# Both feed-forward layers' first product by seven half-size products on two PSUM banks, with the first layer's combined weights made during tile 0

## The reference: what is computed

```python
B, H, S, D = 8, 8, 576, 64                 # q, k, v: (B, H, S, D)
k_p = k.reshape(B, H, S // 8, 8, D).mean(axis=3)      # 72 pooled keys
v_p = v.reshape(B, H, S // 8, 8, D).mean(axis=3)
attn = softmax((q @ k_p.T) / sqrt(D))
x = (attn @ v_p) laid out as (4608 tokens, 512)
h = x @ w1_in;  g = max(0.01 * h, h);               x1  = g @ w1_out
h = x1 @ w2_in; g = h * clip(h + 3, 0, 6) / 6;      out = g @ w2_out
```

## Time and profile before

| | |
|---|---|
| Time, median of 3 runs | 1769.86 us (1765.23 to 1772.93) |
| Profiled execution, its own time | 1768.24 us |
| Its span, first to last instruction | 1766.4 us |
| TensorE busy | 1723.9 us, 98% |
| VectorE, ScalarE, GpSimd busy | 896.7, 634.2, 487.8 us |
| Mean granted TensorE clock | 0.987 of full speed |
| Moved by DMA | 255.41 MB |

### The profile page before, as it was taken

How to read it: one execution, slowest core, us unless ns; L and a number is a source line. 1 busy time by engine, 2 the same in 40 slices (tenths; PEclk the granted TensorE clock), 3 DMA queues, 4 the chain that set the end, 5 groups by cost and what they waited for, 6 DMA issues and landing times.

```text
span 1766.4 us, 28990 instructions
## 1 busy us (share of the span) xinstructions
PE 1723.9 (98%) x9642; PEld 1484.3 (84%) x9642; DVE 896.7 (51%) x1498; ACT 634.2 (36%) x1161; POOL 487.8 (28%) x620
## 2 busy tenths in 40 slices
PE   7899999999999999999999799999999999999999
PEld 7787888888888888888888688998989989898898
DVE  8655555555554655653242345454545454544444
ACT  3544333333333333333222324343434333333332
POOL 7553221222221221213986413030303021121200
PEclk7899999999999999999999899999999999999999
DMA  5332122121121121214557976666756565757562
GB/s 173 112 120 76 47 66 77 45 89 61 38 87 59 63 65 45 76 45 138 189 189 255 337 275 199 198 213 187 220 177 220 178 222 173 224 173 225 174 196 76
DMA packets 141548, 255.41 MB, mean 145 GB/s; under 512 B 14528, under 2 KB 22720, under 8 KB 141504
## 3 DMA queue, kind: packets, MB, share of 16 engines
q1 hardware_dynamic: 141504, 254.86, 44.9%
HBM read 203.42 MB, written 51.38 MB: 144 GB/s over the span
## 4 chain that ended last, share of the span: by engine, by line
PE 79%; POOL 6%; DVE 6%; DMA 3%; ACT 2%; issue 2%; SPq 2%; DVEq 0%; POOLq 0%; ACTq 0%
PE ps_h L1245 14%; PE ps_y L1181 13%; PE ps_y L1183 12%; PE ps_y L1182 12%; PE ps_att L1245 6%; PE ps_h L1181 5%; PE ps_h L1183 5%; PE ps_h L1182 5%; POOL prep_stage L694 2%; PE ps_att L1181 2%; DMA prep_raw<-in_moe_w_out 2%; PE ps_att L1182 2%; PE ps_att L1183 2%; POOL prep_sum L682 2%; POOL prep_stage L692 1%
## 5 line engine op out<-in xcount | busy, mean ns | idle before, releaser
L1245 PE MATMUL ps_h<-xs_hi,ring 128*128 128x256 f32 x1440 | 301.6, 280 | 4.1 <-DMA ring<-w_in_split 3.3
L1245 PEld LDWEIGHTS ps_h<-xs_hi,ring 128*128 128x128 f32 x1440 | 240.4, 188 | 16.9 <-DMA ring<-w_in_split 3.7
L1181 PE MATMUL ps_h<-x_hi,win_hi 128*128 128x512 f32 x576 | 232.3, 403 | 6.3 <-DVE gate L997 6.3
L1181 PE MATMUL ps_y<-wout_hi,g_hi 128*128 128x512 f32 x576 | 227.0, 394 | 3.5 <-issue 3.5
L1181 PE MATMUL ps_y<-g_hi,wout_hi 128*128 128x512 f32 x576 | 229.2, 398 | 0.0
L1183 PE MATMUL ps_y<-wout_hi,g_lo 128*128 128x512 f32 x576 | 227.5, 395 | 0.0
L1183 PE MATMUL ps_h<-x_hi,win_lo 128*128 128x512 f32 x576 | 227.1, 394 | 0.0
L1182 PE MATMUL ps_h<-x_lo,win_hi 128*128 128x512 f32 x576 | 226.6, 393 | 0.0
L1183 PE MATMUL ps_y<-g_hi,wout_lo 128*128 128x512 f32 x576 | 225.9, 392 | 0.0
L1182 PE MATMUL ps_y<-wout_lo,g_hi 128*128 128x512 f32 x576 | 225.6, 392 | 0.0
L1182 PE MATMUL ps_y<-g_lo,wout_hi 128*128 128x512 f32 x576 | 225.0, 391 | 0.0
(11 more groups left out here) (134 smaller groups left out, 3144.1 us busy)
## 6 DMA issues: line engine op xcount, KB each, us to landing
ring<-w_in_split SPq DMA_DIRECT2D x504, 256.0 KB, 2.7
w_in_split<-prep_stage SPq DMA_DIRECT2D x56, 256.0 KB, 2.0
k_raw<-in_kT SPq DMA_DIRECT2D x32, 288.0 KB, 2.9
q_raw<-in_qT SPq DMA_DIRECT2D x32, 288.0 KB, 3.8
v_raw<-in_v SPq DMA_DIRECT2D x32, 288.0 KB
x0T<-x_stage SPq DMA_DIRECT2D x32, 288.0 KB, 2.1
x1T<-y_stage SPq DMA_DIRECT2D x36, 256.0 KB, 2.2
x_stage<-x1T SPq DMA_DIRECT2D x36, 256.0 KB, 3.7
```

Source lines behind the costliest of these rows:

```text
L1181: pe.matmul(acc, left[0], right[0], start=first, stop=False)
L1245: mm = pe.matmul(banks[BANK_OF[r]], a, b[:, r, c, :], start=r < 3 and c == 0 and n == 0, stop=c == 1 and n == 2, skip_group_check=True)
```

## The change

Layer 1's first product is made as layer 2's: seven products of half size per step, the factors of w1_in streamed through the same 14-slot ring in tiles 1 to 8. All 18 tiles (`ALL_TILES`) use one step form, and the first step of layer 2 follows on the last of layer 1; part of each tile's second product runs in the next tile. The seven products use two banks instead of three, in the order A11, S2, A12, S3, S1, A22, S4, so the copies and sums of one product must be done before a product two or three later opens or adds to the same bank.

Layer 1's gate is one DVE instruction that reads `h` twice from SBUF; ACT's `pre` is gone there. ACT copies 2 of a step's blocks and DVE makes 5 sums of 256 columns, in layer 1 as in layer 2. The sums and low parts of x are made on POOL in both layers.

The first layer's factors are made in tile 0, block i + 1 in step i (block 0 before it): the sums and low parts on POOL, the high parts on ACT, straight into the ring, from where SP stores them (`w1_in_split`) for the tiles after. `first_sums` and `last_x_part` make the first tile's x from the four units' results. w1_out is loaded in 8 pieces whose low parts (`piece_lo`) POOL makes in tile 0, too. In tiles 7 and 8 POOL makes 16 split rows of w2_out (`split_row`), three blocks of w2_in factors, tile 8's x, and the other five blocks, and SP stores them between its ring loads.

The order of the seven products, their banks, and the places (8 for each of a tile's 8 steps) of the attention stages in a tile:

```diff
-BANK_OF = (0, 1, 2, 0, 1, 1, 2)
+UNIT_PLACES = [(0, 3, 4, 5, 6, 9, 11, 12, 14),
+               (11, 15, 16, 17, 18, 20, 23, 24, 26),
+               (23, 27, 28, 29, 30, 33, 35, 36, 38),
+               (35, 39, 40, 41, 42, 44, 47, 48, 50)]
...
+A11, S2, A12, S3, S1, A22, S4 = range(PRODUCTS)
+B11, T2, B21, T3, T1, NT4, B22 = range(PRODUCTS)
+BANK_OF = (0, 1, 0, 1, 0, 1, 0)
+OPENS = (0, 1, 4)
...
+        banks = (ps_h[:, 0, 0:HN], ps_h[:, 1, 0:HN])
```

SyncE: tile 0, where each combined factor is stored as it is made; the loop of tiles 1 to 6; tile 7, where `rows_then_factors` stores one row of `w2_out` or one combined factor of `w2_in` at each call:

```diff
+            for i in range(HF):
+                for n in range(PRODUCTS):
+                    if i < HF - 1:
+                        store_factor(i + 1, n)
+                    if i >= HF - 2:
+                        q = PRODUCTS * i + n
+                        sp.wait_ge(ring_stored[q % RING], 16 * USES)
+                        stream(0, i, n, w1_in_split, w1_in_split)
+                    attention_at(0, HF * i + n)
+                attention_at(0, HF * i + PRODUCTS)
+                if 0 < i < HF - 2:
+                    load_raw(i + 2)
...
+            def attention_tile(T, next_unit=True):
+                for i in range(HF):
+                    for m in range(HF):
+                        for r in before_place(m):
+                            stream(T, i, r, w1_in_split, w1_in_split)
+                        attention_at(T, HF * i + m, next_unit)
+                    if i == 1:
+                        store_y(T - 1, False)
...
+            row = n = 0
+            T = ATT_TILES
             for i in range(HF):
                 for r in range(PRODUCTS):
+                    stream(T, i, r, w1_in_split, w1_in_split)
+                    if r < (2, 5, 5, 6, 6, 6, 5, 2)[i]:
+                        row, n = rows_then_factors(1, row, n)
+                if i == 0:
+                    load_x_tile(x0T, T + 1, T + 1)
```

GpSimd: the order of its whole work after the start:

```diff
+            factors(0)
+            first_sums()
+            factors(1)
             sum_unit(1, 0)
+            piece_lo(0)
+            piece_lo(1)
             sum_k(1, 1, 16)
+            factors(2)
             sum_v(1, 1, 18)
+            piece_lo(2)
+            piece_lo(3)
             sum_k(1, 2, 20)
+            factors(3)
+            factors(4)
             sum_v(1, 2, 22)
+            piece_lo(4)
+            piece_lo(5)
             sum_k(1, 3, 24)
+            factors(5)
+            piece_lo(6)
+            piece_lo(7)
             sum_v(1, 3, 26)
+            factors(6)
+            sum_k(2, 0, 28)
+            factors(7)
+            sum_v(2, 0, 30)
+            split_x(1)
+            with pool.Fori(1, ATT_TILES - 1) as T:
+                for c in range(1, PAIRS):
                     sum_unit(T + 1, c)
+                sum_unit(T + 2, 0)
+                split_x(T + 1)
+            for c in range(1, PAIRS):
+                sum_unit(ATT_TILES, c)
+            split_x(ATT_TILES)
             for e in range(FC):
+                split_row(e)
+            for i in range(3):
+                factors2(i)
+            split_x(ATT_TILES + 1)
+            for i in range(3, HF):
+                factors2(i)
+            with pool.Fori(TILES, ALL_TILES) as T:
+                split_x(T)
```

GpSimd: the low parts of one block of first-layer factors, made into the ring that TensorE reads; `factors(i)` is four sums and this:

```diff
+            def factors_lo(i):
+                for n, k in enumerate(PREP_ORDER):
+                    slot = ring_slot(PRODUCTS * i + k)
+                    pool.wait_ge(prep_hi_ready, PRODUCTS * i + n + 1)
+                    nc.gpsimd.tensor_tensor(slot[:, 2:4], factor_source(raw[:, i % 2], k),
+                                            slot[:, 0:2].bitcast(F32), ALU.subtract
+                                            ).then_inc(prep_ready, 1)
```

ScalarE: one step (`place(m)` runs the attention stages of that place, and in tile 0 one high part `factor_hi(i + 1, m)`, which for the sums waits for GpSimd):

```diff
+                act.wait_ge(product_done, PRODUCTS * s + 1)
+                above_zero(act, c21_ready, s)
+                nc.scalar.activation(p1[:], banks[0], ACT.Copy).then_inc(p1_ready, 1)
+                if i == 1 and not is_first(T):
+                    copy_y(T - 1, 0)
+                if i > 0 or not is_first(T):
+                    g_hi_of(s - 1, (i - 1) % HF, 0, before if i == 0 else layer)
+                place(0)
+                act.wait_ge(product_done, PRODUCTS * s + 3)
+                above_zero(act, gate_ready, 2 * s)
+                nc.scalar.activation(h[:, 0, 0:HN], banks[0], ACT.Copy).then_inc(c11_ready, 1)
+                if i == 1 and not is_first(T):
+                    copy_y(T - 1, 2)
+                next_x(0)
+                place(1)
+                next_x(1)
+                place(2)
+                next_x(2)
+                place(3)
+                next_x(3)
+                place(4)
+                if layer == 2:
+                    pre_of(s, 1)
+                g_hi_of(s, i, 1, layer)
+                next_x(4)
+                place(5)
+                next_x(5)
+                place(6)
+                if layer == 2:
+                    pre_of(s, 0)
+                place(7)
+                next_x(6)
```

VectorE: the first layer's gate, and one step:

```diff
+                    nc.vector.scalar_tensor_tensor(gate[:, upper], h[:, upper], SLOPE,
+                                                   h[:, upper], ALU.mult, ALU.max
+                                                   ).then_inc(gate_ready, 1)
...
+                dve.wait_ge(product_done, PRODUCTS * s + 2)
+                dve.wait_ge(p1_ready, s + 1)
+                above_zero(dve, c12_ready, s)
+                add(u2[:], 1, p1[:]).then_inc(u2_ready, 1)
+                if i > 0 or not is_first(T):
+                    last = before if i == 0 else layer
+                    gate_of(s - 1, 0, last)
+                    if is_first(T) and i == 1:
+                        dve.wait_ge(x0_stored[PAIRS - 1], 16)
+                    g_lo_of(s - 1, (i - 1) % HF, 0, last)
+                if i == 1 and not is_first(T):
+                    copy_y(T - 1, 1)
+                place(0)
+                place(1)
+                dve.wait_ge(product_done, PRODUCTS * s + 4)
+                above_zero(dve, c22_ready, s)
+                add(u3[:], 1, p1[:]).then_inc(u3_ready, 1)
+                if i == 1 and not is_first(T):
+                    copy_y(T - 1, 3)
+                place(2)
+                dve.wait_ge(product_done, PRODUCTS * s + 5)
+                dve.wait_ge(u3_ready, s + 1)
+                above_zero(dve, gate_ready, 2 * s - 1)
+                add(h[:, 1, HN:N], 0, u3[:]).then_inc(c22_ready, 1)
+                place(3)
+                dve.wait_ge(product_done, PRODUCTS * s + 6)
+                add(h[:, 1, 0:HN], 1, p1[:]).then_inc(c21_ready, 1)
+                gate_of(s, 1, layer)
+                place(4)
+                dve.wait_ge(product_done, PRODUCTS * s + 7)
+                dve.wait_ge(u2_ready, s + 1)
+                above_zero(dve, gate_ready, 2 * s)
+                add(h[:, 0, HN:N], 0, u2[:]).then_inc(c12_ready, 1)
+                place(5)
+                g_lo_of(s, i, 1, layer)
+                place(6)
+                place(7)
```

TensorE: what a product (`part`) waits for, and one step (`lagging(back, upper, j)` is a quarter, three 512-column matmuls, of the second product of the step `back` before):

```diff
+                if is_first(T):
+                    pe.wait_ge(prep_ready, PRODUCTS * i + PREP_AT[r] + 1)
+                else:
+                    pe.wait_ge(ring_loaded[q % RING], 16 * (USES * (T - 1) + q // RING + 1))
+                if i == 0 and is_first(T):
+                    first_x_ready(r)
+                elif i == 0:
+                    pe.wait_ge(x_ready, PRODUCTS * (T - 1) + r + 1)
...
+                    pe.wait_ge((p1_ready, u2_ready, c11_ready, u3_ready, c22_ready)[r - 2], s + 1)
...
+                part(T, i, 0)
+                part(T, i, 1)
+                lagging(2, 0, 2)
+                place(0)
+                part(T, i, 2)
+                lagging(2, 0, 3)
+                place(1)
+                part(T, i, 3)
+                lagging(1, 1, 0)
+                place(2)
+                part(T, i, 4)
+                lagging(1, 1, 1)
+                place(3)
+                part(T, i, 5)
+                lagging(1, 1, 2)
+                place(4)
+                part(T, i, 6)
+                lagging(1, 1, 3)
+                place(5)
+                lagging(1, 0, 0)
+                place(6)
+                lagging(1, 0, 1)
+                place(7)
```

More of the change, by code:

```diff
@@ L935, in stage, with step, place @@
                                          ACT.Copy, scale=V_SCALE).then_inc(x0_copied, 1)
-            def tile(T, attention, last=False, pieces={}):
-                for place in range(4 * FC):
-                    if place % 4 == 1:
-                        chain(T, place // 4)
+            def step(T, i, layer, before=None, attention=False, turns=True):
+                s = HF * T + i
+                before = before or layer
+                opened = is_first(T) and i == 0
+                def place(m):
@@ L1004, in copy_y, with gate_of @@
[L1004 to L1014 removed]
+            def gate_of(s, upper, layer):
@@ L1079, in spread, with add @@
+            def add(to, bank, other):
+                return nc.vector.tensor_tensor(to, banks[bank], other, ALU.add)
             def spread(per_row):
```

1310 lines of the change are left out of this document (609 added, 701 removed), and 4 rows, old and new, of the table FIRST_STAGES.

## The result

The changed kernel takes 1833.1 us (median of 4 runs, 1829.6 to 1834.7) against 1770.6: ratio 1.0355, 95% interval 1.0327 to 1.0383. It is 59 us above the forecast and outside its range. The page, part 1, to be read against the earlier trace rows: TensorE is busy 2.8 us longer than before and idle 62 us longer; GpSimd is busy 198 us longer.

What follows compares the result with a forecast made beforehand. TensorE, busy 98% of the span, sets the time. Tile 1's start 181, attention tiles 644.4, eleven tiles 924 plus 2.2, seam 10, leftover second product 6.8 and tail 3.4 give 1771.8; with 1.84 outside, 1774 us, range 1748 to 1794.

Steps and rivals of the forecast that it cites:

- The products and the two banks: Layer 2 and other tiles without attention: 84.0 us per tile, 3.3 us gained; two banks cost about 2.2 us over 11 tiles.
- Tiles 1 to 6: Attention tiles: 102.8 us of TensorE work plus 2.0 and 2.6 of waits, 107.4 us each, 644.4 in all.
- The sign that was named for the lock: Layer 1's gate on VectorE, contending with GpSimd for SBUF, would average above 0.75 us in the profile.
- Rivals 1: Attention tiles wait no more than now, 1.3 us: 104.1 us per tile, total 1754 us; chance 0.27.
- rival 2: Attention tiles: GpSimd's SBUF work blocks VectorE's gate, 4.8 us per tile instead of 2.6; 109.6 us, total 1787; chance 0.19.
- Tile 0: First tile hangs on GpSimd's in-order list of 117.9 us plus 2.1 of waits; tile 1 starts at 181 us.
- The forecast's own sign of being wrong: In the first tile: wrong if GpSimd does not bound it; POOL was expected busy over 90% before tile 1.
- Tiles 7 and 8: Two tiles of 84.0 us around the layer change plus a seam of 10 us, bounds 0 and 20, instead of 18.6.
- rival 3: At the seam, tile 7's excess DMA isn't absorbed and late rows delay tile 8's x: seam 20, total 1784; chance 0.12.
- there the loads for layer 2 hide under the products: In tile 8, 32 MB of DMA traffic just fits, so layer 2's loads hide under the products.
- The two ends: Tile 1's start, 181 us with bounds 173 and 190, and the seam, 10 us with bounds 0 and 20.
- the middle: The six attention tiles between first tile and seam: 107.4 us each, 644.4 us together.

## Why the prediction was wrong

**The products and the two banks: right, but for the turn.** A layer-2 tile takes 84.95 us, not 84.0. The two banks cost nothing (three give 84.95 too). The forecast laid out ACT's copy of p in mid-tile and found 1 us to spare "while ACT is free then"; at the turn ACT has the next tile's xs_hi ahead of it, and that is 0.4 to 0.5 us a tile. Of the other half, 8 x 0.03 us lie in the steps (10.53 each instead of 10.50) and as much still at the turn (10.74); what makes them stays open. The whole term was 2.2 us for 11 tiles, and in the nine of them behind the seam it measured 776.5 - 756 - 6.8 - 3.4 = 10.3, of which 1.2 is tile 9 (86.2), which begins at the lower clock (0.67 in its first 5 us).

**Tiles 1 to 6: right in the sum, 644.7 against 644.4, and partly by luck.** From 236 to 772.8 us TensorE is busy 104.4 us per tile, where its own work was put at 102.8, and idle 3.0, where 4.6 was added for waits: the two parts miss by 1.6 us each, in opposite directions. Of the waits one was tested: GpSimd's low parts at the turn cost 1.25 us of the 2.6 given to GpSimd. How the rest of the 107.4 divides between ACT's copies, VectorE and pooling isn't shown; the order of one copy on ACT changed nothing. The sign that was named for the lock is there: the gate takes 776 ns on average, above 0.75 us. Rivals 1 (104.1) and 2 (109.6) are both out, in these tiles.

**Tile 0: the step that failed, 33.6 us.** "From there tile 0 hangs on GpSimd, whose list is in order": the sum of its list, 117.9, was right to 2 us, and it was taken for the time. A list is only the bound if it never waits. This one is in a ring of waits with ACT (high parts), SyncE (raw blocks behind a v load that waits for GpSimd again) and TensorE (steps that free ring slots and banks), so a delay of any one comes round to all. The forecast gave ACT's high parts 2.1 us and the DMAs nothing. GpSimd stood idle for 37.2: 10.6 + 6.4 behind ACT's high parts, 13.3 behind raw blocks, 3.3 behind the load of x, the rest in small pieces. The forecast's own sign of being wrong came up: GpSimd is busy 76% of the tile (115.8 of 153 us), not over 90%. Shown by experiment: tile 1 starts 10.2 us earlier with the raw loads asked for early in SyncE's list, 27.9 earlier with the low parts of w1_out left out as well, 20.5 with them on VectorE. That the four lists hold each other up is how these numbers and the waits are read; why ACT's high parts and x are still late with both edits, where GpSimd stands idle for 20.9 us, stays open. The lock of rival 2 struck here, not in the attention tiles where the rival priced it: one gate of 6.22 us.

**Tiles 7 and 8: the second step, 17.6 us.** The bytes were counted and gave 9.3 us of excess, and rival 3 named the mechanism (late rows delay x of tile 8) and put it at 20. The seam measured 27.6. Missing was what full DMA engines do to a chain: GpSimd has four rows in flight, each took up to 11 us to land instead of the 2 us GpSimd needs for one, so it waited 14.1 + 4.7 us in a list that filled 81.6 of the tile's 84. Rows stored twice (+17.5) and halved (-7.8) show the bytes. The order on GpSimd alone gives 1.6. With both, 9.3 us are gone, and the wait left, 9.1 us at the start of tile 9, is for a ring load issued behind the loads of w2_out: "there the loads for layer 2 hide under the products" is not borne out, and in the changed kernel the lateness of tile 8 covers most of it.

**The chances.** The two ends were taken as independent of the middle and small (173 to 190, 0 to 20). Both came out above their upper bounds, by 214.6 - 190 = 24.6 and 27.6 - 20 = 7.6 us, together over half the miss.

## What to carry to other kernels

Before a list's sum of busy time is taken as the length of a stage, ask for each item what it waits for, and whether that comes round to the list itself; where four engines pass blocks in a ring, the waits can be large (here 37 us beside 116 of work), and two suspects are to be tested together as well as alone, since each can hide the other. Of a stage with full DMA queues, cost the latency of its small loads as well as its bytes: two more rows in flight, free in memory, and an earlier first load gave 1% where a redesign of the products lost 3.5%. An eighth less arithmetic is only worth what the waits leave of it.

## What the runs showed of the hardware

- VectorE's gate with both inputs in SBUF took 6.22 us for 0.69 of work, from 102.90 to 109.12, beside two GpSimd subtractions of 2.4 and 2.3 us and the first k pooling behind them, which follow each other without a gap up to 108.6. In the Trainium skill, "SBUF — State Buffer", section "Summary: rules for kernel authors", a VectorE instruction with two SBUF inputs beside a GpSimd one that reads SBUF blocks fully, if it is the second to issue, until the first finishes; the trace agrees that it blocks, but it was held past more than one instruction. With zeros written in place of the two subtractions no gate of tile 0 took over 1.32 us.
- One wait of 10.7 us of TensorE is followed by a product at 1.62 us instead of 0.71, with the granted clock at 0.50; so a wait in tile 0 costs more than its length. TensorE is busy 107.7 us from 62 to 215 at a mean clock of 0.85, and 103.5 us with both edits of tile 0, from 62 to 187 at 0.91.
- A 256 KB row asked for between 878 and 901 us takes 7.6 to 11.1 us from issue to landing, with the DMA share at 1.04 (393 GB/s); the loads of raw blocks in tile 0, from 102 us on, take 2.2 to 3.9 us each, where the share is 0.56 from 120 to 215. A ring load behind four loads of w2_out takes 12.4.
